# Routing beside the expert products: list work on VectorE with one operand in PSUM, low parts moved from GpSimd to VectorE, a new order of work

## The reference

```python
    cap = N // E
    logits = x @ w_gate
    order = np.argsort(-logits.flatten())
    for idx in order:
        tok, e = (int(idx) // E, int(idx) % E)
        if assigned[tok] >= 0 or counts[e] >= cap:
            continue
        assigned[tok] = e
        counts[e] += 1
    for e in range(E):
        mask = assigned == e
        h = np.maximum(x[mask] @ w1[e], 0.0)
        out[mask] = h @ w2[e]
```

## Time and profile before

| | |
|---|---|
| median of 3 runs | 1429.39 us (1427.9 to 1437.05) |
| the profiled execution | 1429.68 us, span 1427.9 us |
| busy: PE, DVE, ACT, POOL | 88%, 44%, 23%, 33% of the span |
| mean granted TensorE clock | 0.92 of full speed |

### The profile page before, as it was taken

How to read it: one execution, slowest core, us unless ns; L and a number is a source line. 1 busy time by engine, 2 the same in 40 slices (tenths; PEclk the granted TensorE clock), 3 DMA queues, 4 the chain that set the end, 5 groups by cost and what they waited for, 6 DMA issues and landing times.

```text
span 1427.9 us, 21801 instructions
## 1 busy us (share of the span) xinstructions
PE 1256.5 (88%) x7790; PEld 1129.0 (79%) x7790; DVE 622.7 (44%) x1472; ACT 322.0 (23%) x675; POOL 466.1 (33%) x380
## 2 busy tenths in 40 slices
PE   3667789999999999999999999999459789788886
PEld 2566669999999999999999999999448678677776
DVE  6666652222222222222222256667686665664321
ACT  2434421111111111111111111111022234133352
POOL 4656581000330000700002500000055676568673
PEclk9888899999999999999999999999657888879798
DMA  6676751000110000200000100000132232233220
GB/s 247 186 213 187 202 139 34 0 0 0 36 53 0 0 0 0 77 11 0 0 0 0 44 22 22 22 22 22 60 124 73 77 116 77 72 94 103 85 91 27
DMA packets 35441, 90.63 MB, mean 63 GB/s; under 512 B 4944, under 2 KB 14544, under 8 KB 35280
## 3 DMA queue, kind: packets, MB, share of 16 engines
q1 hardware_dynamic: 31184, 77.62, 17.9%
q0 software_dynamic: 3072, 9.44, 2.0%
q10 hardware_dynamic: 1152, 3.15, 0.6%
HBM read 71.31 MB, written 9.44 MB: 57 GB/s over the span
## 4 chain that ended last, share of the span: by engine, by line
PE 69%; DVE 8%; POOL 6%; issue 3%; ACT 1%; DMA 0%; POOLq 0%; ACTq 0%; DVEq 0%
PE ps L961 22%; PE ps L963 21%; PE ps L962 21%; PE ps L1027 2%; DVE ge L787 2%; DVE onehot L797 2%; POOL out L508 2%; DVE at_least L823 1%; POOL w_lo L513 1%; POOL h_lo L536 1%; POOL xs L524 1%; DVE low L791 1%; POOL xg L519 1%; PE ps L1042 1%; PE ps L919 0%
## 5 line engine op out<-in xcount | busy, mean ns | idle before, releaser
L961 PE MATMUL ps<-w_hi,h_hi 128*128 128x384 f32 x960 | 335.3, 349 | 10.3 <-POOL h_lo L536 10.3
L695 DVE SCALAR_TENSOR_TENSOR h_lo<-ps,h_hi 128x512 fp32r<-128x512 f32 x192 | 132.7, 691 | 474.8 <-ACT h_hi L374 474.6
L963 PE MATMUL ps<-w_hi,h_lo 128*128 128x384 f32 x960 | 330.0, 344 | 0.0
L962 PE MATMUL ps<-w_lo,h_hi 128*128 128x384 f32 x960 | 329.2, 343 | 0.0
L961 PE MATMUL ps<-xs,w_hi 128*128 (+1 forms) x768 | 303.0, 395 | 5.3 <-POOL xs L524 2.1
L963 PE MATMUL ps<-xs,w_lo 128*128 (+1 forms) x768 | 298.0, 388 | 0.0
L962 PE MATMUL ps<-xs,w_hi 128*128 (+1 forms) x768 | 297.8, 388 | 0.0
L374 ACT ACTIVATE h_hi<-ps 128x512 fp32r<-128x512 f32 x192 | 115.2, 600 | 685.3 <-PE ps L963 685.3
L431 POOL TENSOR_TENSOR w_hi<-w_raw,zero_t 128x768 fp32r<-128x768 f32 x32 | 46.9, 1467 | 504.9 <-PE ps L963 504.9
L961 PEld LDWEIGHTS ps<-w_hi,h_hi 128*128 128x128 f32 x960 | 185.6, 193 | 19.4 <-POOL h_lo L536 12.6
L962 PEld LDWEIGHTS ps<-w_lo,h_hi 128*128 128x128 f32 x960 | 186.0, 194 | 6.2
(11 more groups left out here) (155 smaller groups left out, 1188.9 us busy)
## 6 DMA issues: line engine op xcount, KB each, us to landing
w_raw<-experts SPq DMA_DIRECT2D x88, 384.0 KB, 3.0
rkv<-rkv_tok SPq DMA_DIRECT2D x24, 576.0 KB, 4.8
rk<-rk_t SPq DMA_DIRECT2D x24, 512.0 KB, 4.1
xs<-y_parts SPq DMA_DIRECT2D x48, 144.0 KB, 3.5
x_rows<-x_tok SPq DMA_DIRECT2D x6, 768.0 KB, 3.5
w_raw<-experts ACTq DMA_DIRECT2D x8, 384.0 KB, 8.9
xs<-y_parts SPq DMA_DIRECT2D x16, 96.0 KB, 2.5
wg_b<-w_gate_rows SPq DMA_DIRECT2D x1, 1536.0 KB, 6.2
```

The lines of the kernel that those rows point to most:

```text
L695: eng.scalar_tensor_tensor(out=h_lo[:, f % SLOTS, :], in0=ps[:, 4 + f % SLOTS, :], scalar=0.0, in1=h_hi[:, f % SLOTS, :].bitcast(fp32), op ...
L961: eng.matmul(out, a_hi, b_hi_, start=first, stop=False)
L962: eng.matmul(out, a_hi, b_lo_, start=False, stop=False)
L963: return eng.matmul(out, a_lo, b_hi_, start=False, stop=last)
```

## The change

- In almost every DVE instruction of the routing that reads two tensors, one is put into PSUM (spare columns of banks 3 and 7): candidates, preferences, `row`, `raw`, `code`, `mine`, `tied`, `total`, `lower_key`, `low`, and copies of constants. `taken` gets a copy in PSUM.
- `place` has another form (`past`, `blk`, `low`, three instructions for `rhs`) and `spots` is one instruction for a range of tiles in place of one for each.
- `h_lo` is made by DVE out of PSUM (`low_part`), placed by hand between the routing's steps; `hf` and ACT's second relu go. PE waits for `m_lo` in place of `m_full`.
- Weight tiles are taken four ahead (`LOOK`) in place of three: the next slot's tiles 0 to 3 come behind tiles 4 to 7.
- POOL's order is new: weight tile 4, the scatter of the slot before, tile 5, `idx_o`, tiles 6 and 7, the next slot's tiles 0 to 3, then the gather and `rows` for the next slot. In the last slot POOL also makes `w_lo`, which DVE did before.
- `assign` is cut into `close`, `again`, `settle` and `remove`, and these run at the end of a slot: `ties(s + 1)` stands before part 38 and `ranks(s + 1)` after part 42, `place` and `spots` run ahead of the search, `numbers(s)` stands after part 9.
- The products of slot 0 begin after three steps of the search for slot 1, not after all six.

```diff
+LOOK = 4
@@ scalar, slot
-                    eng.wait_ge(m_lo, s * FT + f + (2 if f < 2 else 1))
-                    eng.activation(h_hi[:, f % SLOTS, 0:CAP], ps[:, 4 + f % SLOTS, 0:CAP], ACT.Relu)
-                    eng.activation(hf[:, f % SLOTS, :], ps[:, 4 + f % SLOTS, 0:CAP], ACT.Relu).then_inc(m_full, 1)
-                    if f + 3 < FT:
-                        weights(s, f + 3)
+                    eng.activation(h_hi[:, f % SLOTS, 0:CAP], ps[:, 4 + f % SLOTS, 0:CAP], ACT.Relu).then_inc(m_full, 1)
+                    if f + LOOK < FT:
+                        weights(s, f + LOOK)
                     elif not final:
-                        weights(s + 1, f + 3 - FT)
+                        weights(s + 1, f + LOOK - FT)
@@ gpsimd, slot
-                for f in range(FT):
-                    if f == 1:
-                        if not isinstance(s, int) or s > 0:
-                            eng.wait_ge(o_out, s * (16 * QB))
-                        eng.tensor_tensor(idx_o[:], idx[:], zero_i[:].to_broadcast([P, QB]), ALU.add).then_inc(r_cp, 1)
-                    eng.wait_ge(m_full, s * FT + (SLOTS + f + 1))
-                    eng.tensor_tensor(h_lo[:, f % SLOTS, 0:CAP], hf[:, f % SLOTS, :], h_hi[:, f % SLOTS, 0:CAP].bitcast(fp32),
-                                      ALU.subtract).then_inc(m_lo, 1)
-                    if not final and f + 3 < FT:
-                        weights(s, f + 3)
-                    elif not final and not to_final:
-                        weights(s + 1, f + 3 - FT)
-                    if not final and f == 4:
-                        gather(s + 1, [(p_tk, 2 * s + 1)])
+                weights(s, LOOK)
+                if not first:
+                    scatter(s - 1, 2 * s)
+                weights(s, LOOK + 1)
+                if not first:
+                    eng.wait_ge(o_out, s * (16 * QB))
+                eng.tensor_tensor(idx_o[:], idx[:], zero_i[:].to_broadcast([P, QB]), ALU.add).then_inc(r_cp, 1)
+                for f in range(LOOK + 2, FT):
+                    weights(s, f)
                 if not final:
+                    for f in range(LOOK):
+                        weights(s + 1, f)
+                    gather(s + 1, [(p_tk, 2 * s + 1)])
                     for c in range(KC):
                         rows(s + 1, c)
-                    scatter(s, 2 * s + 2)
@@ vector
+            def low_part(s, f):
+
+                eng.wait_ge(m_full, s * FT + (SLOTS + f + 1))
+                eng.scalar_tensor_tensor(out=h_lo[:, f % SLOTS, 0:CAP], in0=ps[:, 4 + f % SLOTS, 0:CAP], scalar=0.0,
+                                         in1=h_hi[:, f % SLOTS, 0:CAP].bitcast(fp32), op0=ALU.max, op1=ALU.subtract).then_inc(m_lo, 1)
@@ place and spots
-                step(eng.tensor_tensor(ge[:], pos[:].unsqueeze(1).to_broadcast([P, QB + 1, TILES]),
-                                       bounds[:].unsqueeze(2).to_broadcast([P, QB + 1, TILES]), ALU.is_ge))
-                eng.tensor_tensor(part[:], ge[:, 0:QB, :], ge[:, 1:QB + 1, :], ALU.subtract)
+                eng.tensor_scalar(far, pos[:], 512.0, None, ALU.add)
+                step(eng.tensor_scalar(past, pos[:], float(P - 512), None, ALU.is_ge))
+                step(eng.scalar_tensor_tensor(out=blk[:], in0=pos[:], scalar=float(2 * P - 512), in1=past, op0=ALU.is_ge, op1=ALU.add))
+                step(eng.scalar_tensor_tensor(out=low, in0=blk[:], scalar=-float(P), in1=far, op0=ALU.mult, op1=ALU.add))
+                for a in range(QB):
+                    eng.scalar_tensor_tensor(out=rhs[:, :, a, :], in0=blk[:].unsqueeze(2).to_broadcast([P, TILES, 2]), scalar=float(a),
+                                             in1=jp.rearrange("p (j z) -> p j z", z=2), op0=ALU.is_equal, op1=ALU.mult)
-                for j in range(first, end):
-                    o = eng.tensor_scalar(onehot[:, j, :], iota_b, low[:, 1, j:j + 1], None, ALU.is_equal)
+                here = slice(first, end)
+                o = eng.tensor_tensor(onehot[:, here, :], low[:, here].unsqueeze(2).to_broadcast([P, end - first, P]),
+                                      iota_b.unsqueeze(1).to_broadcast([P, end - first, P]), ALU.is_equal)
@@ order of DVE in a slot
+            def around(s):
+
+                place(s)
+                spots(0, 18)
+                low_part(s - 1, 0)
+                spots(18, TILES)
+                low_part(s - 1, 1)
+                find(s + 1, 0)
+                low_part(s - 1, 2)
+                judge(s + 1, 0)
+                number(s)
+                find(s + 1, 1)
...
+                judge(s + 1, 5)
+                close(s + 1)
+                low_part(s - 1, 6)
@@ order of PE in a slot
+            STEADY = [(3, 1), (3, 1), (2, 1), (4, 1), (2, 1), (3, 1)]
+            def around(s):
+
+                products(s - 1, 0, 10)
+                numbers(s)
...
+                products(s - 1, at_part, TURNED - 1)
+                ties(s + 1)
+                products(s - 1, TURNED - 1, TURNED)
+                gathered(s, 0)
+                gathered(s, 1)
+                products(s - 1, TURNED, TURNED + KC)
+                gathered(s, 2)
+                products(s - 1, TURNED + KC, TURNED + KC + 1)
+                ranks(s + 1)
+                products(s - 1, TURNED + KC + 1, 2 * FT * KC)
```

More of the change, by code:

```diff
@@ L121, in layered_mixture_kernel @@
         pos = new("pos", [P, TILES])
[L122 to L125, removed]
+        blk = new("blk", [P, TILES])
         rhs = new("rhs", [P, TILES, QB, 2], bf16)
@@ L686, in _ @@
             eng.memset(minus[:], -1 / P)
[L687 to L690 removed]
+            step(eng.memset(taken_p, 0.0))
+            step(eng.memset(taken[:], 0.0))
             def low_parts(n, between=None):
@@ L837, in assign, with find @@
-            def assign(s, last=False):
+            def find(s, t):
+                k = WIDTHS[t]
+                key, skip = (upper_key, key2)[t >= 3], k % 2
+                cands = first_c[:, t // 3, 1:1 + k] if t % 3 == 0 else narrow[:, skip:skip + k]
+                if t > 0:
+                    eng.wait_ge(r_c, s * STEPS + t)
+                if t == 3:
+                    step(eng.scalar_tensor_tensor(out=key2[:], in0=upper_key[:], scalar=narrow[:, 0:1], in1=lower_key, op0=ALU.subtract, op1=ALU.add))
+                for half in range(2):
+                    here = slice(half * JH, (half + 1) * JH)
+                    eng.tensor_tensor(at_least[:, here, 0:k], key[:, here].unsqueeze(2).to_broadcast([P, JH, k]),
+                                      cands.unsqueeze(1).to_broadcast([P, JH, k]), ALU.is_ge).then_inc(r_ge, 1)
@@ L882, in _ @@
-            place(E2 - 2)
-            spots(0, TILES)
+            for t in range(STEPS):
+                find(0, t)
+                judge(0, t)
+                if t == 0:
+                    eng.tensor_copy(jp, jp_b)
+            eng.wait_ge(x2_out, 16 * NTB)
+            close(0)
+            again()
+            settle(0)
+            remove()
+            place(0)
+            spots(0, TILES)
+            find(1, 0)
+            judge(1, 0)
+            number(0)
+            for t in range(1, 4):
+                find(1, t)
+                judge(1, t)
@@ new lines, in _ @@
+            find(1, 4)
+            low_part(0, 0)
+            judge(1, 4)
+            find(1, 5)
+            low_part(0, 1)
+            judge(1, 5)
+            close(1)
+            low_part(0, 2)
+            again()
+            settle(1)
+            low_part(0, 3)
+            remove()
+            place(1)
+            spots(0, JH)
+            low_part(0, 4)
+            spots(JH, TILES)
+            find(2, 0)
+            low_part(0, 5)
+            judge(2, 0)
+            number(1)
@@ new lines, in _ @@
+            find(2, 1)
+            judge(2, 1)
+            find(2, 2)
+            low_part(0, 6)
+            judge(2, 2)
+            find(2, 3)
+            low_part(0, 7)
+            judge(2, 3)
+            for t in range(4, STEPS):
+                find(2, t)
+                judge(2, t)
+            close(2)
+            again()
+            settle(2)
+            remove()
+            start = done[0]
+            around(2)
+            again()
+            settle(3)
+            low_part(1, 7)
@@ new lines, in _ @@
+            remove()
+            PER = done[0] - start
+            with eng.Fori(3, E2 - 3) as s:
+                done[0] = s * PER + (start - 2 * PER)
+                around(s)
+                again()
+                settle(s + 1)
+                low_part(s - 1, 7)
+                remove()
+            done[0] = start + PER * (E2 - 5)
+            around(E2 - 3)
+            settle(E2 - 2)
+            low_part(E2 - 4, 7)
+            remove(last=True)
+            place(E2 - 2)
+            spots(0, 18)
```

260 lines of the change are left out of this document (145 added, 115 removed).

## The result

| | before | changed |
|---|---|---|
| median | 1429.72 us (10 runs) | 1443.28 us (10 runs) |
| ratio | | **1.0091**, 95% interval 1.0071 to 1.011 |
| profiled execution, its span | 1429.68 us, 1427.9 us | 1438.33 us, 1436.5 us |
| mean granted clock | 0.92 | 0.92 |

A rewrite of the whole routed layer comes out 0.9% slower. The measured time is inside the range of 1412 to 1455 us, but just above the forecast's own part of it (1420 to 1443), and nearer to the rival of a longer half clock (1450) than to the forecast. One of the ten executions of the kernel before took 4635 us, and the ratio goes by the other nine (1424 to 1438 us).

The account below looks back on a forecast made before the run. PE bounds the kernel; in the routed layer it loses time to waits for DVE and POOL and to the clock. A steady slot was 35.6 + 9.3 + 2.9 + 1.2 = 49.0 us against 49.1; forecast 1433 us, range 1412 to 1455.

Parts of the forecast that it names:

- rival of a longer half clock: Behind the gather's gaps the clock returns only after 10.8 us, 2.5 us more in each of seven slots: 1450 us, chance 0.27.
- The bound and the gain: In the routed slots, one operand in PSUM ends DVE's wait for POOL; PE's 7.5 us gap (4.6 in other slots) goes.
- DVE still waits for POOL: Rival: `place` is still held for up to 7.5 us and five slots pay 6 us: 1463 us, chance 0.05.
- The gather: Late in POOL's queue, it leaves PE an uncovered gap ahead of the transposes, 9.3 us in each of slots 0 to 6.
- The gather is covered after all: Rival: the gaps before the transposes and their clock vanish, 7 x 12.2 us: 1348 us, chance 0.06.
- The clock behind it: Behind each gather's gap PE runs at half clock for a while, costing 2.9 us.
- `idx_o` behind the scatter: On POOL, `idx_o` done at 11.4 us after a slot's start delays DVE's `number`; PE loses 1.2 us in slots 1 to 4.
- clock nearly free: Rival: the slow stretch is used up inside the gather's gaps, 7 x 2.9 us come back: 1413 us, chance 0.12.
- The start: Before slot 0, POOL's four weight tiles precede the first gather; the first product starts at 1050.1 us, 7.6 us earlier.
- Slot 0 and slot 1: First two routed slots: slot 0 predicted at 64.7 us, including half clock of 5.0 and 2.9; slot 1 at 50.5 us.
- Slot 5: Slot without a search: 28.0 us, gap and clock 12.2, and `ranks(7)` waiting 2.8 us for `idx_o`; 43.0 us predicted.
- The low parts: Moved to DVE, they relieve POOL of 8 x 1.0 us a slot, end PE's 1.3 us wait, and cost nothing.

Follow-up runs that it names:

- e5: Changed kernel with the routing operands it had put in PSUM (matmul outputs excepted) in SBUF: 1475.13 us, 1.0213 of the kernel before.
- e6: e1 with the routing operands in SBUF in place of PSUM (matmul outputs excepted): 1416.70 us, 0.9822 of the kernel before.
- e9: Kernel before in its own order, with the changed kernel's routing instructions alone (PSUM operands, new `place` and `spots`): 1402.08 us, 0.9713 of the kernel before.
- e1: Changed kernel with POOL issuing the next slot's gather ahead of that slot's weight tiles 0 to 3: 1376.93 us, 0.9538 of the kernel before.
- e2: Kernel before with POOL's gather moved from behind f = 4 to the slot's end: 1509.80 us, 1.0445 of the kernel before.
- e3: Changed kernel with the gather between the next slot's weight tiles 2 and 3: 1415.00 us, 0.9789 of the kernel before.
- e4: Changed kernel with 72 useless matmuls filling PE's gap ahead of the transposes of slots 1 to 7: 1424.45 us, 0.9862 of the kernel before.
- e10: Changed kernel with 24 useless narrow matmuls ahead of `ranks(1)` and 24 ahead of `numbers(1)`: 1436.06 us, 0.9944 of the kernel before.
- e8: e1 with the low parts back on POOL and ACT's second relu with them: 1388.07 us, 0.9604 of the kernel before.
- e7: e1 with scatter and `idx_o` earlier on POOL, ranks and last transposes two parts later, slot 0's parts respread: 1359.94 us, 0.9416 of the kernel before.

## Why the prediction came out as it did

**The bound and the gain: right.** Where one operand lay in PSUM, DVE's wait for POOL was gone; no comparison went over 945 ns. "DVE still waits for POOL" is out, but for `left`, whose operands both stayed in SBUF. e5 and e6 put the gain at 33 to 41 us, e9 at 44 us in the old order, with the new forms of `place` and `spots`.

**The price of a PSUM operand: nothing, as taken.** 756 elements take 934 and 940 ns from PSUM after, 941 to 949 from SBUF before where nothing held them up. By the table of the Trainium skill ("VectorE: DVE Perf Modes", TRN2 errata), 120 cycles against 58, it would be 65 ns more for each, an estimate; these rows don't show them.

**The gather: right.** "Sum 9.3 us, in each of the slots 0 to 6": 9.02, 9.19, 9.34, 9.54, 9.26, 9.03 and 9.08 us. e1, e2 and e3 show its cause from three sides. "The gather is covered after all" is out.

**The clock behind it: right, a little dear.** I took 2.9 us; the half clock lasted 4.0 to 5.3 us after the steady gaps, so 2.0 to 2.7 us each. The rival of a longer half clock is out: even behind slot 0's gap it lasted 7.5 us, and its mark was 9. e4's 17 us agree with these in sum, and rule out the clock nearly free as well.

**`idx_o` behind the scatter: right in time, wrong in price.** It was done 10.9 us after the start of slots 2 and 3 (predicted 11.4), but PE lost 0.5 us a slot in slots 2 to 4, not 1.2. With the clock's 2.0 to 2.7 us in place of 2.9, hence 48.0 us for the steady slot in place of 49.0.

**The start: 1.5 us late.** The fourth `w_lo` ended 34.3 us after the keys, not 33.0.

**Slot 0 and slot 1: the terms that were mis-sized.** "Half clock at its start 5.0 and behind the gap 2.9" left out a second fall, 14.15 us at half clock (7.1 us) ahead of the gap and 7.53 us (3.8 us) behind it. It came behind two waits of 1.36 and 1.23 us that I had forecast myself (3.1 us) and priced without their clock; e10 shows that without them it does not come. Other terms of the slot were too large by some 2 us in all, so it was 70.2 us for 64.7. In slot 1 a wait of 2.0 us ahead of a count and 6.8 us at half clock (3.4 us) stand in place of 1.2 us: 53.8 for 50.5.

**Slot 5: mis-sized.** `ranks(7)` waited 5.49 us, not 2.8, and the clock fell for 6.8 us (3.4 us) behind that: 47.3 for 43.0.

**Together:** +1.5, +5.5, +3.3, three times -1.0, +4.3, and nothing at the end: 422.2 predicted, 433.6 measured. The dense layers of that execution were 5 us shorter, which is why the profiled 1438.3 us lies nearer to the forecast than the stage does. The likeliest case won by its mechanism, not by its time: the 1443.3 us lie nearer to the 1450 of a rival that the traces rule out. The sign of the small difference (0.9%) was inside what I had called no change. The error is mostly of one kind: small waits were counted for their length and not for the half clock behind them, which is some 15 us (7.1 and 0.9 in slot 0, 3.4 each in slots 1 and 5), while two lengths were 3.5 us short; terms that were too large hide the rest. On another chip the changed kernel was even with before (0.9987), since before loses 13.6 us there and the changed kernel 2.

**The low parts: right that POOL is relieved, at a value I had not worked out.** e8 puts it at 14 us behind an early gather, nearly all of it in the last three slots.

## What to carry to other kernels

When an instruction is put behind a queue of others, follow what releases the last of them: here the queue ended in an instruction that waits for PE itself, and PE's next item waited for the queue. A large rewrite that "does nothing" can be a gain and a loss of the same size; moving one call told them apart (1.009 on the first chip and 0.999 on another with the call late, 0.954 with it early). Price a wait of over a microsecond on PE at its length and then at its length with the clock that may fall behind it, and look in slots that are not steady first: three of this kernel's eight held all of the error.

## What the runs showed of the hardware that was not expected

**Short waits can be enough for the clock.** In slot 0 of the changed kernel PE stood still for 1.36 and 1.23 us, with 5.6 us of work between, and the granted clock went to 0.50 1.8 us after the second. With both filled it stayed at 1.00 (e10). One such wait can do as well. In slot 0 of e7 the first of the two is 0.33 us and the second 1.30 us; the clock fell 1.6 us behind the second and was at 0.50 for 13.6 us. Nor does such a wait always bring a fall. In e7 waits of 1.11 and 1.12 us in slots 2 and 3 left the clock at 1.00, and 1.15 us at the same place in slot 4 did not; in slot 0 of e8 it stayed at 1.00 behind 1.56 us. What decides was not tried and stays open.

**A DVE instruction can wait through several of POOL's.** `ge` of the earlier trace rows started at 1215.81. POOL's instructions then followed each other without a break, five of 1.0 to 1.8 us, the last of them from 1221.56 on for 1.79 us, so until 1223.35. `ge` ended at 1223.48.

**PE's updates can come late beside indirect DMAs.** An update is the semaphore signal by which PE tells another engine that a result is there. In e1, the timelines of PE, POOL and DVE; the count's last matmul ends at about 1206.46, and DVE, idle, takes it up at 1208.24. POOL issues indirect DMAs meanwhile:

```profile
1205.70 0.76 PE L1134 MATMUL ps<-pref,at_least 128*31 128x8 bf16 x24
...
1208.46 0.30 PE L1148 MATMUL ps<-passed,units 63*128 63x1 bf16 x3 [1.27 <-issue]
```

```profile
1205.43 0.99 POOL L523 DMA_INDIRECT xg<-x_rows,idx  x1 [0.16 <-issue]
1206.72 0.96 POOL L523 DMA_INDIRECT xg<-x_rows,idx  x1 [0.30 <-issue]
```

```profile
1208.24 0.15 DVE L833 TENSOR_SCALAR_CACHE_REDUCE okays<-ps 31x8 bf16<-31x8 f32 x1 [2.68 <-remote]
```

I counted PE's updates that came over 0.85 us after the start of the matmul that gives them, from 1000 us on: 1 in before and 0 in the changed kernel on the first chip; 11 and 16 when both were run again, 31 in e1, 10 to 18 in most other runs, but 3 in e2 and 2 in e5. By a narrower count, which takes the last such matmul ahead of each update, there are 155 in all traces together, and every one has an indirect DMA of POOL beside it (between the start of its matmul and the update, or within 0.3 us of that); in e1 these DMAs fill 47 us of the stage's 364. That is a coincidence in time in every case; no run moved the DMAs alone to show the cause. In the kernel before, run again, PE's waits (from 1057 us on) show what has grown:

```profile
PE ps L1027 <- DVE at_least L823: 31.8, 6, 7.5
...
PE ps L1042 <- DVE okays L828: 8.0, 6, 1.7
```

The first was 27.7 us in the earlier trace rows, and the second occurred once on the first chip, with 1.7 us. Together they are 10.4 us more, and with the clock behind them they can hold the 13.6 us. Only the second is what was expected of that run: DVE judges a count late there, since the update of that count comes 1.4 to 2.5 us after the start of its matmul. The first grew because the wait behind `place` was 7.5 us in slots 2 and 4, where it had been 4.6 us, and what sets that length is not shown. Why the first chip is nearly free of late updates, and e2 and e5 on other chips too, was not tried and stays open.
